# Transposes instead of identity products, and 64-row products with zero-filled gap rows, in a fused linear-attention and mixture-of-experts kernel

## What is computed

```python
# B, H, S, D = 4, 8, 768, 48
state = zeros((B, H, D, D))
for t in range(S):
    cur = einsum('bhd,bhe->bhde', u[None] * k[t], v[t])
    y[:, :, t] = einsum('bhd,bhde->bhe', r[t], state + cur)
    state = w[None, :, :, None] * state + einsum('bhd,bhe->bhde', k[t], v[t])
x = y.transpose(0, 2, 1, 3).reshape(B * S, H * D)      # 3072 x 384
```

## Time and profile before

| | |
|---|---|
| median of 3 runs | 302.24 us (301.41 to 302.4) |
| profiled execution | 301.77 us, its span 300.0 us |
| TensorE's busy share | 93%, 277.9 us |
| VectorE, ScalarE, GpSimd | 54%, 24%, 21% |
| mean granted TensorE clock | 0.968 |
| HBM traffic | 47.56 MB read, 4.72 MB written |

### The profile page before, as it was taken

One profiled execution on the slowest core, in us unless ns is written; L12 is line 12 of the kernel. 1 busy time (PEld: TensorE's weight loads), 2 busy tenths in 40 slices (PEclk: granted clock), 3 DMA queues, 4 the chain that ended last, 5 costly groups with the idle time before them and its releaser, 6 DMA issues.

```text
span 300.0 us, 11059 instructions
## 1 busy us (share of the span) xinstructions
PE 277.9 (93%) x4821; PEld 237.5 (79%) x4821; DVE 161.8 (54%) x293; ACT 72.0 (24%) x150; POOL 62.3 (21%) x67
## 2 busy tenths in 40 slices
PE   8688399999999999999999989999999999999992
PEld 8576288888888788864334968999999999999992
DVE  5956428787878888753340238643352433525312
ACT  1002013223322332241102316323222222222200
POOL 3725205544564475050000000000000000000000
PEclk9959859999999999999999999999999999999998
DMA  5966926999999999887894090002020020200203
GB/s 150 250 137 211 294 82 204 302 347 258 332 276 320 340 271 367 289 309 309 306 418 174 8 391 23 2 1 105 0 95 10 0 105 0 105 0 0 105 3 110
DMA packets 13957, 52.57 MB, mean 175 GB/s; under 512 B 2032, under 2 KB 5296, under 8 KB 12144
## 3 DMA queue, kind: packets, MB, share of 16 engines
q1 hardware_dynamic: 12928, 41.28, 44.0%
q10 hardware_dynamic: 1008, 11.01, 9.4%
HBM read 47.56 MB, written 4.72 MB: 174 GB/s over the span
## 4 chain that ended last, share of the span: by engine, by line
PE 83%; DVE 4%; issue 3%; DMA 2%; ACT 1%; SPq 1%; DVEq 0%
PE ps L1094 11%; PE ps L1093 11%; PE ps L1095 11%; PE ps L885 10%; PE ps L865 6%; PE ps L876 5%; PE ps L837 4%; PE ps L1078 4%; PE ps L965 4%; PE ps L988 4%; PE ps L844 3%; PE ps L855 3%; PE ps L890 3%; DMA wraw<-wb 2%; DVE rkb L574 2%
## 5 line engine op out<-in xcount | busy, mean ns | idle before, releaser
L1094 PE MATMUL ps<-w2l,hh 128*128 128x384 f32 x192 | 64.5, 336 | 0.0
L1093 PE MATMUL ps<-w2h,hh 128*128 128x384 f32 x192 | 64.4, 336 | 0.0
L1095 PE MATMUL ps<-w2h,hl 128*128 128x384 f32 x192 | 64.3, 335 | 0.0
L753 DVE SCALAR_TENSOR_TENSOR hl<-ps,hh 128x512 fp32r<-128x512 f32 x48 | 32.9, 690 | 57.3 <-ACT hh L513 57.2
L513 ACT ACTIVATE hh<-ps 128x512 fp32r<-128x512 f32 x48 | 28.5, 598 | 74.7 <-PE ps L1078 74.7
L403 POOL TENSOR_TENSOR rk<-ind 112x512 f32<-112x512 f32 x24 | 30.9, 1287 | 55.1 <-PE ps L844 45.2
L1094 PEld LDWEIGHTS ps<-w2l,hh 128*128 128x128 f32 x192 | 36.0, 188 | 1.7
L1093 PEld LDWEIGHTS ps<-w2h,hh 128*128 128x128 f32 x192 | 36.0, 188 | 0.6
L1095 PEld LDWEIGHTS ps<-w2h,hl 128*128 128x128 f32 x192 | 36.1, 188 | 0.0
L574 DVE TENSOR_TENSOR rkb<-ind,tab 112x1024 f32<-112x1024 f32 x24 | 33.4, 1392 | 0.2
L885 PE MATMUL ps<-ident,xs 112*128 112x112 f32 x200 | 30.5, 299 | 0.0
(11 more groups left out here) (159 smaller groups left out, 347.3 us busy)
## 6 DMA issues: line engine op xcount, KB each, us to landing
wearly<-wa ACTq DMA_DIRECT2D x7, 1536.0 KB, 8.8
intk<-tmaj SPq DMA_DIRECT2D x24, 384.0 KB, 6.9
ind<-dmaj SPq DMA_DIRECT2D x44, 192.0 KB, 7.3
wearly<-wa SPq DMA_DIRECT2D x4, 1536.0 KB, 10.5
out<-acc SPq DMA_DIRECT2D x5, 768.0 KB, 3.5
wlate<-wa SPq DMA_DIRECT2D x4, 768.0 KB, 5.1
wlate<-wa SPq DMA_DIRECT2D x2, 1536.0 KB, 8.7
wmid<-wa SPq DMA_DIRECT2D x1, 1536.0 KB, 6.5
```

The lines of the kernel that those rows point to most:

```text
L753: v.scalar_tensor_tensor(out=hl[:, f % 4, :], in0=ps[:, f % 4, :], scalar=0.0, in1=hh[:, f % 4, :].bitcast(F32), op0=ALU.max, op1=ALU.subt ...
L1093: mm(o, a_h, w2h[:, f, :], start=(f == 0), stop=False)
L1094: mm(o, a_h, w2l[:, f, :], start=False, stop=False)
L1095: ins = mm(o, a_l, w2h[:, f, :], start=False, stop=(f == KF - 1))
```

## The change

1. `turn` calls `nc.tensor.transpose` on the same operands instead of `matmul`.
2. `scores` and `carried` take their operands over `toks[j]` (64 rows) instead of `rows[j]` (48 rows). For that the gap rows must hold zeros or harmless values: `u` and the last column of the table are zero there (`wusb[:, 1]` set to 0, two small seed tiles made on GpSimd), `w` is 1 there, and rows 48 to 63 and 112 to 127 of each of the four `ind` slots are filled once with data by two new transfers of 16 rows per slot. All operations on `0:R2` now cover 128 partitions.
3. New waits: SyncE's first transfer waits for VectorE's two fills of `wusb` (`zeroed`), VectorE waits for 12 instead of 7 constants of GpSimd before it starts the table, and both `pre(0)` and GpSimd's first `rk` wait for `gap_in` at 8 x 16, which is all eight new transfers.

```diff
@@ SyncE
             def load_d(n):
                 src = dmaj[...]
-                low = HB if n < 4 else D
-                sp.dma_start(ind[0:low, n % 4, :, :], src[:, 0:low, 0:2]).then_inc(ind_in[n % 4], 16)
+                if n < 4:
+                    sp.dma_start(ind[D:HB, n % 4, :, :], src[:, 0:HB - D, 0:2]).then_inc(gap_in, 16)
+                    sp.dma_start(ind[R2:P, n % 4, :, :], src[:, 0:HB - D, 0:2]).then_inc(gap_in, 16)
+                sp.dma_start(ind[0:D, n % 4, :, :], src[:, 0:D, 0:2]).then_inc(ind_in[n % 4], 16)
                 sp.dma_start(ind[HB:R2, n % 4, :, :], src[:, D:2 * D, 0:2]).then_inc(ind_in[n % 4], 16)
...
-            sp.dma_start(wusb[0:HB, :, :], wu[0:HB]).then_inc(wu_in, 16)
+            sp.wait_ge(zeroed, 1)
+            sp.dma_start(wusb[0:D, :, :], wu[0:D]).then_inc(wu_in, 16)
             sp.dma_start(wusb[HB:R2, :, :], wu[D:2 * D]).then_inc(wu_in, 16)
@@ GpSimd: rk
                 pool.wait_ge(ind_in[slot], (n_ // 4 + 1) * 32)
+                if n_ == 0:
+                    pool.wait_ge(gap_in, 8 * 16)
                 wait(pool, sc_done, n_ - 1)
-                g.tensor_tensor(rk[0:R2, k2, :], ind[0:R2, slot, 0, :], ind[0:R2, slot, 1, :],
+                g.tensor_tensor(rk[:, k2, :], ind[:, slot, 0, :], ind[:, slot, 1, :],
@@ VectorE
+            v.memset(wusb[:, 0, :], 1.0)
+            v.memset(wusb[:, 1, :], 0.0).then_inc(zeroed, 1)
...
+            dve.wait_ge(consts, NCONST)
+            link(v.tensor_tensor(seed[:, :], seed[:, :], seed2[:, :], ALU.add))
+            v.tensor_copy(tab[:, :, 1, HALF - 1:HALF], seed[:, 0:1].unsqueeze(1).to_broadcast([P, PAIRS, 1]))
...
             def pre(n):
                 dve.wait_ge(ind_in[n % 4], (n // 4 + 1) * 32)
+                if n == 0:
+                    dve.wait_ge(gap_in, 8 * 16)
@@ TensorE: scores, carried, turn
-                        mm(ps[toks[m], SC + j, B * HALF:2 * B * HALF], ubc[rows[j], ip, :],
-                           rk[rows[j], ip % 2, :]...
+                        mm(ps[toks[m], SC + j, B * HALF:2 * B * HALF], ubc[toks[j], ip, :],
+                           rk[toks[j], ip % 2, :]...
...
-                            ins = mm(ps[toks[m], SC + j, b * HALF:(b + 1) * HALF], rkb[rows[j], ip, 1, at_],
-                                     rkb[rows[j], ip, 0, at_], start=True, stop=True, skip_group_check=True)
+                            ins = mm(ps[toks[m], SC + j, b * HALF:(b + 1) * HALF], rkb[toks[j], ip, 1, at_],
+                                     rkb[toks[j], ip, 0, at_], start=True, stop=True, skip_group_check=True)
...
-                    ins = mm(ps[:, TB, b * P:b * P + R2], xs[0:R2, b, :], ident[0:R2, 0:R2], start=True, stop=True)
+                    ins = nc.tensor.transpose(ps[:, TB, b * P:b * P + R2], xs[0:R2, b, :], ident[0:R2, 0:R2])
```

More of the change, by code:

```diff
@@ L107, in mixed_kernel @@
         winv = sb("winv", [P, PAIRS])
+        seed = sb("seed", [P, 1])
+        seed2 = sb("seed2", [P, 1])
         phisb = sb("phisb", [P, 2, PAIRS, NS])
@@ L173, in mixed_kernel @@
         tok_in = [sem(f"tok_in{i}") for i in range(4)]
+        gap_in = sem("gap_in")
         dch = sem("dch")
@@ L271, in mixed_kernel @@
         PARTS = ((0, 1), (1, 3), (3, 6))
-        NCONST = 7
+        NCONST = 12
         NCONST2 = NCONST + 1 + 7
@@ L295, in _ @@
             load_t(1)
-            sp.wait_ge(zeroed, 1)
+            sp.wait_ge(zeroed, 2)
             for i in range(2):
@@ L388, in _ @@
             step(g.memset(xs[:, :, :], 0.0))
+            step(g.memset(seed[:, :], 1.0))
+            step(g.memset(seed2[:, :], 1.0))
             pool.wait_ge(consts, n[0])
+            step(g.affine_select(out=seed[:, :], in_=seed[:, :], compare_op=ALU.is_gt, fill=0.0,
+                                 base=D, pattern=[[0, 1]], channel_multiplier=-1))
+            step(g.affine_select(out=seed2[:, :], in_=seed2[:, :], compare_op=ALU.is_gt, fill=0.0,
+                                 base=1 - HB, pattern=[[0, 1]], channel_multiplier=1))
+            pool.wait_ge(consts, n[0])
+            step(g.affine_select(out=seed2[:, :], in_=seed2[:, :], compare_op=ALU.is_gt, fill=0.0,
+                                 base=R2, pattern=[[0, 1]], channel_multiplier=-1))
             step(g.affine_select(out=strict[:, :], in_=ones[:, :], compare_op=ALU.is_gt, fill=0.0,
@@ L564, in _ @@
-            link(v.reciprocal(winv[0:R2, :], pw[0:R2, 5, :]))
+                scale = pw[0:P, i, :].unsqueeze(2).to_broadcast([P, PAIRS, m])
+                v.tensor_tensor(tab[0:P, :, 0, m:2 * m], tab[0:P, :, 0, 0:m], scale, ALU.mult)
+                v.tensor_tensor(tab[0:P, :, 1, HALF - 2 * m:HALF - m], tab[0:P, :, 1, HALF - m:HALF], scale, ALU.mult)
+                link(v.tensor_tensor(pw[0:P, i + 1, :], pw[0:P, i, :], pw[0:P, i, :], ALU.mult))
+            link(v.reciprocal(winv[0:P, :], pw[0:P, 5, :]))
@@ L572, in pre @@
                 wait(dve, y_done, n - 3)
-                tab_ = tab[0:R2, n % PAIRS, :, :].unsqueeze(2).to_broadcast([R2, 2, 2 * B, HALF])
-                v.tensor_tensor(rkb[0:R2, n % 4, :, :].rearrange("p i (g t) -> p i g t", t=HALF),
-                                ind[0:R2, n % 4, :, :].rearrange("p i (g t) -> p i g t", t=HALF), tab_,
+                tab_ = tab[0:P, n % PAIRS, :, :].unsqueeze(2).to_broadcast([P, 2, 2 * B, HALF])
+                v.tensor_tensor(rkb[0:P, n % 4, :, :].rearrange("p i (g t) -> p i g t", t=HALF),
+                                ind[0:P, n % 4, :, :].rearrange("p i (g t) -> p i g t", t=HALF), tab_,
@@ L576, in pre @@
                                 ALU.mult).then_inc(pre_ready, 1)
-            half = pw[0:R2, 5, :].unsqueeze(2).to_broadcast([R2, PAIRS, HALF])
-            v.tensor_tensor(wk[0:R2, :, 0, :], tab[0:R2, :, 1, :], half, ALU.mult)
-            v.tensor_tensor(wk[0:R2, :, 1, :], tab[0:R2, :, 1, :], half, ALU.mult).then_inc(wk_ready, 1)
+            half = pw[0:P, 5, :].unsqueeze(2).to_broadcast([P, PAIRS, HALF])
+            v.tensor_tensor(wk[0:P, :, 0, :], tab[0:P, :, 1, :], half, ALU.mult)
+            v.tensor_tensor(wk[0:P, :, 1, :], tab[0:P, :, 1, :], half, ALU.mult).then_inc(wk_ready, 1)
@@ L599, in update @@
                 def update(out, old, m):
-                    inc = ps[0:R2, SB + m, 0:B * D].rearrange("p (b d) -> p b d", b=B)
-                    return v.scalar_tensor_tensor(out=out, in0=old, scalar=pw[0:R2, 6, ip:ip + 1], in1=inc,
+                    inc = ps[0:P, SB + m, 0:B * D].rearrange("p (b d) -> p b d", b=B)
+                    return v.scalar_tensor_tensor(out=out, in0=old, scalar=pw[0:P, 6, ip:ip + 1], in1=inc,
                                                   op0=ALU.mult, op1=ALU.add).then_inc(st_ready, 1)
@@ L605, in _ @@
                 wait(dve, st_ready, 2 * (n - PAIRS) + 2 + 1 if c else 0)
-                update(stb[0:R2, ip, :, :], sta[0:R2, ip, :, :], 0)
+                update(stb[0:P, ip, :, :], sta[0:P, ip, :, :], 0)
                 dve.wait_ge(sc_done, n + 1)
@@ L615, in _ @@
                 dve.wait_ge(car_done, n + 1)
-                update(sta[0:R2, ip, :, :], stb[0:R2, ip, :, :], 1)
+                update(sta[0:P, ip, :, :], stb[0:P, ip, :, :], 1)
                 if n + 2 < STEPS:
@@ L836, in scores @@
                     for m in range(2):
-                        mm(ps[toks[m], SC + j, B * HALF:2 * B * HALF], ubc[rows[j], ip, :],
-                           rk[rows[j], ip % 2, :].rearrange("p (b m t) -> p m b t", b=B, m=2)[:, m],
+                        mm(ps[toks[m], SC + j, B * HALF:2 * B * HALF], ubc[toks[j], ip, :],
+                           rk[toks[j], ip % 2, :].rearrange("p (b m t) -> p m b t", b=B, m=2)[:, m],
                            start=True, stop=True, skip_group_check=True)
@@ L864, in carried @@
                         st = stb if m else sta
-                        ins = mm(ps[rows[j ^ b % 2], YB + m, b * HALF:(b + 1) * HALF], st[rows[j], ip, b, :],
-                                 rkb[rows[j], ip, 0, b * C + m * HALF:b * C + (m + 1) * HALF],
+                        ins = mm(ps[rows[j ^ b % 2], YB + m, b * HALF:(b + 1) * HALF], st[toks[j], ip, b, :],
+                                 rkb[toks[j], ip, 0, b * C + m * HALF:b * C + (m + 1) * HALF],
                                  start=(swap and b < 2), stop=False, skip_group_check=True)
```

15 lines of the change are left out of this document (5 added, 10 removed).

## The result

| | before | changed |
|---|---|---|
| median (17 runs each, same chip) | 302.4 us (300.59 to 305.96) | 305.41 us (301.92 to 308.25) |
| ratio, 95% interval | | 1.0074 (1.0049 to 1.0099) |
| profiled execution, its span | 301.77, 300.0 us | 303.82, 302.0 us |

The changed kernel is slower by 0.7%, where +0.4% was forecast. The sum of the prediction was +1.2 us on the profiled execution; it is +2.05. That these are near each other hides a term that was three times too large, and two that were too small.

What follows compares the result with a forecast made beforehand. TensorE is busy 93%, but expert and step loads fill the DMA engines and set the pace of later steps. 6.9 - 5.5 - 0.2 = +1.2 us on 301.77 profiled, with 0.5 for the median 303.4 us; range 298.3 to 307.0.

Steps and rivals of the forecast that it cites:

- The start: Before step 0: waiting for all eight gap transfers moves pre(0) and the first carried products 9.6 us later.
- The turn itself: TensorE's turn in each step: transposes save 0.5 us warm and 0.95 us cold.
- rival (c): In the turn: transposes no cheaper inside a step, near 311 us, or clock falls, 306.5; chance 0.10 together.
- Steps 0 to 4: First five steps: late start less cheaper turns, plus 0.3 us for a low clock, leaves +6.9 us.
- rival (b): At step 3: the 4.92 us code stall shrinks by up to 4 us, near 300.5 us; chance 0.10.
- 64 rows and 128 partitions: Products over 64 rows, VectorE and GpSimd over 128 partitions: costed at nothing; row passage bounds 0 to 0.07 us per step.
- Steps 5 to 23: Remaining steps: 9.5 us saved if TensorE alone sets them, but only 5.5 of it comes.
- Steps 5 to 7: Steps before the DMA engines fill: they give 1.5 us.
- Steps 8 to 19: DMA-full stretch: bytes set the pace, gain eats about 3 us of load lead; steps 4.0 to 4.2 instead of 4.29 us.
- Steps 20 to 23: Last steps, taken to lie behind the last expert load: they give about 1 us.
- rival (d): Gap transfers land later than their bytes say, or GpSimd and VectorE slow each other: +1.5 to +3, near 306; chance 0.10.
- After the steps: The turn behind the loop, ahead of later TensorE work: saves 0.4 us at most, 0.2 taken.

Runs made afterwards that it cites:

- experiment 3: Changed kernel with one gap semaphore per slot, so pre(n) and rk(n) wait only for their own slot's two gap transfers; 298.74 us, ratio 0.988.
- experiment 4: Kernel before plus the eight gap transfers and the waits for all of them in pre and rk; 312.47 us, ratio 1.0401.
- experiment 1: Kernel before with the turn done by transposes and nothing else changed; 294.47 us against 302.15, ratio 0.9754.
- experiment 5: Kernel before with the seven expert loads issued behind all 24 steps; only steps read, 8 to 20 take 4.19 us instead of 4.28.
- experiment 6: Kernel before with transposes in the turn and the seven expert loads behind all steps; only steps read, 8 to 20 take 3.92 us.
- experiment 9: Kernel before with transposes, expert loads behind the steps, and half of pre from step 4 on; steps 8 to 20 take 3.81 us.
- experiment 10: Kernel before with transposes, expert loads two steps later, and rk a step earlier in four buffers, after pre; 292.08 us, ratio 0.9676.
- experiment 11: Kernel before with transposes, the early four-buffer rk, and expert loads behind the steps; steps 8 to 20 take 3.81 us.
- experiment 7: Kernel before with transposes and expert loads issued after steps 3, 6, ... 21 instead of 1, 4, ... 19; 293.06 us, ratio 0.9664.

## Why the prediction was right, and where it was not

**The start: right.** Forecast +9.6 for the carried products, at 25.7; measured 25.77, +9.72. `pre(0)` came at 17.26 instead of 18.2, and the second `pre` and GpSimd's work took the difference back. (The prediction has 18.1 as its sum and 18.2 right behind it; its 9.6 goes with 18.1.) Experiments 3 and 4 show the reason given, the wait for slots that no early step uses.

**The turn itself: right.** 0.54 saved warm (1.07 to 0.53) and 1.04 cold (1.98 to 0.94), against 0.5 and 0.95. The Trainium skill ("TensorE: Matmul & The Clock Gate", Terms) says four times faster; this trace shows half the time. The same page's section on the PE-mode transpose says that a transpose doesn't count as busy "the same way"; the granted clock of 1.00 over 51.5 us with 0.53 us of transposes in each step shows no loss from that, and rival (c) is out.

**Steps 0 to 4: 1.3 us too dear.** +5.61 at step 5 instead of +6.9. The stall of 4.92 us stayed, as said (4.76, but in two pieces, in steps 2 and 3); rival (b) did not happen. The rest of the difference has no single place that I can show, and whether the 0.3 us for a late clock were spent isn't separated from it.

**64 rows and 128 partitions: right for the steps, open for the whole.** Undisturbed steps take 4.01 us with identity products and 3.73 with transposes, over 48 rows and over 64. But experiment 3 is 1.3% slower than experiment 1, and nothing in the prediction's sum stands for that beside the start.

**Steps 5 to 23: the term that failed.** "Together 5.5 of the 9.5" came out as 1.8 (from +5.61 to +3.80). Its pieces:
- Steps 5 to 7: 1.5 forecast, 0.8 measured.
- Steps 8 to 19: 3 forecast, 3.3 measured, and steps of 4.00 us in the 4.0 to 4.2 given. That the number is right is partly luck. "The bytes alone set the present pace" leaves out a second bound: without the expert loads the old step is still 4.19 us long (experiment 5), and the transposes win the same 0.27 (experiment 6). What held the gain in these steps at 0.28 instead of 0.5 was the loop of experiment 9. The prediction had VectorE's sum, "3.5 us of work in a step that would be 3.7", and took it for the bound that comes next at 3.7; it didn't follow the dependence `scores`, mask, copy, `within`, which gives 3.73 whatever else VectorE has to do.
- Steps 20 to 23: 1 us to win forecast, 2.35 lost, and this is most of the error. The prediction took these steps to lie "behind the last expert load" and to be free. They do not, and the lead of the loads, which it said faster steps would eat, was gone: r, k loads issued between 95 and 110 us land after 11.1 us in the median, against 6.9 in the kernel before. VectorE in order of time in the changed kernel:

```profile
114.90 1.22 DVE L597 TENSOR_TENSOR rkb<-ind,tab 128x1024 f32<-128x1024 f32 x1 [2.21 <-DMA ind<-dmaj]
...
118.41 2.15 DVE L597 TENSOR_TENSOR rkb<-ind,tab 128x1024 f32<-128x1024 f32 x1
...
124.43 1.23 DVE L597 TENSOR_TENSOR rkb<-ind,tab 128x1024 f32<-128x1024 f32 x1 [1.50 <-DMA ind<-dmaj]
```

  The last load of r, k, issued at 110.42, lands at 124.41, and the seventh expert load goes out at 113.29, in the midst of it. Experiment 1 shows the same (4.89 us per step there), experiment 6 without the loads does not (3.81).

The place of this loss is not fixed: experiment 3 has it before step 20 (4.35 us per step from 8 to 20, then 4.08), experiment 10 too (4.21, then 3.93). The sum is steadier. From step 5 to step 23 the five transposing kernels with expert loads take 73.7 to 76.7 us (experiments 10 and 3; the changed kernel 75.10), those without 68.4 to 70.5. The prediction's own 4.27 us per step by the bytes is 76.9 for these 18 steps. So its bound by bytes fits the whole, if the changed kernel ate 1.8 us of lead. What failed is the 5.5: to a lead of 3 us it added 1.5 for steps 5 to 7 and 1 for steps 20 to 23, as if only the steps between had to pay for the bytes.

**VectorE and GpSimd slowing each other**, the second half of rival (d), happened, and not at the start only: `pre` at 1566 ns on average. The rival speaks of work on the same tiles, but that isn't needed: `kt` reads `intk` and `kttab`, `pre` reads `ind` and `tab`. It was sized at +1.5 to +3 in all; experiment 11 gives 0.11 us per step, 2 us in all, in kernels without expert loads.

**After the steps: 0.2 forecast, 1.75 won.** From the last `scores` to the logits' next products (L943, now L966) the chain takes 7.73 us instead of 8.56; 0.55 of that is the last turn, which hides behind nothing. The other 0.9 us come in the later stages, where the change touches nothing, and are less than the spread between runs of one kernel: a group of four expert loads behind attention is issued 2.96 us later than before (at 145.84), the first piece of the output 2.16 later (205.71). Why was not tried.

The sum of what was measured: +9.7 at the start, -4.1 up to step 5, -1.8 up to step 23, -1.75 behind it: +2.05. The forecast was right in sign, but two errors of opposite sign (3.7 too hopeful in the steps, 2.9 too cautious around them) helped it, which is luck.

**The better versions.** The transposes alone (0.975) beat both kernels; with the expert loads moved (0.966, experiment 7) or `rk` moved as well (0.968, experiment 10) the medians are lower still, at 293.06 and 292.08 us, but the intervals of the three overlap.

## What to carry to other kernels

When a piece of the busiest engine's work gets shorter, look for the loop of dependences that doesn't contain it, and measure its length in the trace: that, and not the sum of work of any engine, says how much of the saving can show. A wait for "all" of something costs the latest of them; count the transfers queued ahead of that one, since one semaphore per slot brought back 6 of 9 us. Where loads nearly fill the DMA engines, steps that get faster gain at first from the loads' lead and pay when it is used up. So hold the bytes against the whole loop, not against a stretch in its middle, and check by the issue times which steps are really free of the large loads.

## What the runs showed of the hardware

**VectorE and GpSimd take turns on SBUF.** In the pairs looked at, each with two operands from SBUF, the later one's time grows by about what the other still has to run. In the changed kernel `pre(0)` and `rk(0)` start 0.04 us apart at 17.26; one takes 1.23 us, the other 2.30, where it takes 1.27 alone. Here it is the other way round, GpSimd and VectorE in order of time in the changed kernel:

```profile
60.46 1.00 POOL L426 TENSOR_TENSOR kt<-intk,kttab 128x384 f32<-128x384 f32 x1 [0.36 <-DMA intk<-tmaj]
```
```profile
60.50 2.05 DVE L597 TENSOR_TENSOR rkb<-ind,tab 128x1024 f32<-128x1024 f32 x1
```

The Trainium skill ("SBUF — State Buffer", SBUF: two separate sides) calls the port pair that the two share "an **exclusive lock**, not a bandwidth split", also for a VectorE operation with two SBUF inputs. These rows agree, to within 0.2 us. In the kernel before `pre` already took 1392 ns on average, against 1.22 us alone; the prediction took its durations from single rows and missed the difference.

**TensorE can stand without a releaser while loads fill the queues.** TensorE stood 4.92 us without a releaser while the first 1.5 MB load moved, 1.09 us when that load was taken away, 1.30 when it came later; and an early start meets another such stall in step 1 (3.21 and 3.49 us). In these last two no expert load had been issued yet, and the step loads filled the DMA engines. The prediction read the stall as program code that arrives late. The queues agree in part: two instruction packets moved during the stall of 4.92 us and one during each of 3.21 and 3.49, none during those of 1.09 and 1.30; but none moved either during the second piece in the changed kernel (2.18 us). That it is code is argued, not shown. Where TensorE came earlier to such a stall, most of the gain was lost in it: 0.2 us was left behind the first one in experiment 1.
